# Two heads' short rows beneath one another, one transpose each, and loads of v that wait for ScalarE

## The reference

```
B, H, S, D = 4, 8, 576, 64
scores = matmul(q, k.T) / sqrt(D)                      # per batch and head, 576 x 576
kth    = 32nd largest of each row
attn   = softmax(where(scores >= kth, scores, -1e9))
x      = matmul(attn, v)  -> rows (B*S, H*D) = (2304, 512)

h = x @ w_in; g = max(h, 0) + alpha * min(h, 0); x = g @ w_out     # 512 -> 2048 -> 512

live = x @ w_skip > 0;  e = argmax(x @ w_gate)                     # 8 experts
out  = x;  out[live] = x + gate * (max(x @ w1[e], 0) @ w2[e])      # 512 -> 1024 -> 512
```

## Time and profile before

| what | us |
|---|---|
| time, median of 3 runs | 1122.45 |
| the profiled execution, its time | 1120.2 |
| its span, first to last instruction | 1118.4 |
| DVE busy | 907.7 (81%) |
| PE busy | 924.3 (83%) |
| ACT busy | 631.6 (56%) |
| POOL busy | 427.6 (38%) |

### The profile page before, as it was taken

One profiled execution on the slowest core, in us unless ns is written; L12 is line 12 of the kernel. 1 busy time (PEld: TensorE's weight loads), 2 busy tenths in 40 slices (PEclk: granted clock), 3 DMA queues, 4 the chain that ended last, 5 costly groups with the idle time before them and its releaser, 6 DMA issues.

```text
span 1118.4 us, 22555 instructions
## 1 busy us (share of the span) xinstructions
PE 924.3 (83%) x6271; PEld 616.4 (55%) x6272; DVE 907.7 (81%) x2006; ACT 631.6 (56%) x1324; POOL 427.6 (38%) x598
## 2 busy tenths in 40 slices
PE   5345588898899889988988898889888898399996
PEld 2223356575667566665756576657565666243342
DVE  4899999999999999999999999999999451711110
ACT  3785869637954784588458746964784371110100
POOL 0136647612841483068127702851384000201110
PEclk9986679999999999999999999999999799699999
DMA  7910201004001300220031003100300156735750
GB/s 205 369 34 3 51 22 33 23 2 119 8 21 50 78 0 21 75 53 10 11 96 32 21 1 101 26 22 16 81 1 1 43 191 224 237 100 180 226 197 18
DMA packets 98658, 84.05 MB, mean 75 GB/s; under 512 B 69116, under 2 KB 77308, under 8 KB 98048
## 3 DMA queue, kind: packets, MB, share of 16 engines
q1 hardware_dynamic: 94544, 78.56, 23.3%
q0 software_dynamic: 1488, 3.15, 0.8%
q10 hardware_dynamic: 2528, 1.18, 0.4%
HBM read 72.64 MB, written 11.53 MB: 75 GB/s over the span
## 4 chain that ended last, share of the span: by engine, by line
PE 55%; issue 10%; POOL 10%; ACT 9%; DMA 7%; DVE 5%; SPq 1%; POOLq 1%; ACTq 0%; DVEq 0%
PE acc L607 16%; PE acc L574 8%; PE sc L545 7%; PE acc L593 6%; DMA arena<-in_moe_w_dram 5%; PE pt_full L563 5%; POOL pos_part L361 4%; POOL arena L363 2%; PE sc L715 2%; PE pt_full L775 2%; POOL arena L1330 2%; PE acc L616 2%; ACT arena L847 2%; DVE best L1053 1%; PE acc L622 1%
## 5 line engine op out<-in xcount | busy, mean ns | idle before, releaser
L1053 DVE MAX8 best<-arena 128x8 f32<-128x576 f32 x576 | 403.5, 741 | 9.6 <-issue 5.4
L1066 DVE MATCH_REPLACE8 arena<-best,arena 128x576 f32<-128x576 f32 x432 | 315.8, 738 | 0.0
L1330 POOL TENSOR_SCALAR arena<-arena,row_inv 128x576 f32<-128x576 f32 x144 | 105.5, 750 | 360.0 <-DVE row_inv L1083 360.0
L593 PE MATMUL acc<-arena 128*128 (+1 forms) x1536 | 202.4, 286 | 28.0 <-ACT neg_part L886 26.1
L607 PE MATMUL acc<-arena 128*128 128x288 f16 x1536 | 202.0, 288 | 2.9 <-issue 2.9
L593 PEld LDWEIGHTS acc<-arena 128*128 128x128 f16 x1536 | 146.3, 98 | 78.9 <-issue 39.1
L607 PEld LDWEIGHTS acc<-arena 128*128 128x128 f16 x1536 | 149.5, 99 | 49.5 <-issue 12.9
L563 PE MATMUL pt_full<-ident,arena 128*128 128x128 f32 x576 | 101.9, 305 | 63.8 <-ACT arena L860 31.0
L838 ACT ACTIVATE arena<-sc 128x576 f32<-128x576 f32 x144 | 92.1, 642 | 86.1 <-PE sc L545 69.6
L1071 DVE SCALAR_TENSOR_TENSOR arena<-arena,best 128x576 f32<-128x576 f32 x144 | 128.0, 935 | 3.5 <-ACT arena L847 3.5
L563 PEld LDWEIGHTS pt_full<-ident,arena 128*128 128x128 f32 x576 | 72.7, 154 | 94.0 <-issue 51.0
(11 more groups left out here) (173 smaller groups left out, 942.1 us busy)
## 6 DMA issues: line engine op xcount, KB each, us to landing
arena<-in_moe_w_dram SPq DMA_DIRECT2D x64, 512.0 KB
nat<-in_v_dram SPq DMA_DIRECT2D x64, 128.0 KB, 2.2
nat<-in_k_dram SPq DMA_DIRECT2D x60, 128.0 KB, 2.7
x_rows<-x2n SPq DMA_DIRECT2D x24, 192.0 KB, 2.5
out_dram<-x2n SPq DMA_DIRECT2D x24, 192.0 KB, 2.6
nat<-in_q_dram SPq DMA_DIRECT2D x64, 64.0 KB, 2.1
arena<-in_moe_w_in_dram SPq DMA_DIRECT2D x4, 1024.0 KB, 7.3
arena<-in_moe_w_out_dram SPq DMA_DIRECT2D x4, 1024.0 KB, 13.7
```

The costliest lines, as they stand in the source:

```text
L593: last = nc.tensor.matmul(dst[:, 0:HALF], win16[:, a, d, f * P:(f + 1) * P], xT16[:, bass.ds(row + d, 1), b, :].rearrange("p b s -> p (b s)"),
L1053: nc.vector.max(best[:, gp, j, r, :], src).then_inc(max_found if r == 0 else dve_step, 1)
L1066: nc.vector.match_replace(left[:, j, :], best[:, gp, j, r, :], src, MASKED).then_inc(dve_step, 1)
L1330: nc.gpsimd.tensor_scalar(probs[:, gp, j, :], probs[:, gp, j, :], row_inv[:, gp, j:j + 1], 1.0, ALU.mult, ALU.mult)\
```

## The change

The four short rows of a quad's heads are no longer side by side in 32 (or 64) partitions. The second head pair's rows lie in the partitions beneath the first pair's: `q_rest` becomes 64 partitions of 128 numbers, `k_rest` 128 partitions of 128. One transpose each then gives the same 64 and 128 columns in the same bank. Each of the two loads becomes two DMAs of half the size, one for each head pair, so a pass's q and k come in 12 DMAs and not 10. The semaphore `pv_done`, with TensorE's wait for its own product, is gone; SyncE waits instead until ScalarE has rounded both halves of x of that pass, which it does after it has read the product.

```
-        k_rest = sb("k_rest", [REST, QUAD, D])
+        k_rest = sb("k_rest", [TWO * REST, TWO * D])
...
-        q_rest = arena[0:QREST, at[4]:at[5]].rearrange("p (h d) -> p h d", h=QUAD)
+        q_rest = arena[0:TWO * QREST, at[4]:at[5]]
...
-        DMAS_QK, DMAS_V = 2 * (QUAD + 1), QUAD + 1
+        DMAS_QK, DMAS_V = 2 * (QUAD + TWO), QUAD + 1
...
-            engine.dma_start(k_rest[:, :, :], quad_of(k, p)[:, FULL * P:S, :].rearrange("h r d -> r h d")).then_inc(qk_loaded, 16)
+            for c in range(TWO):
+                engine.dma_start(k_rest[c * REST:(c + 1) * REST, :].rearrange("r (h d) -> r h d", d=D),
+                                 quad_of(k, p)[2 * c:2 * c + 2, FULL * P:S, :].rearrange("h r d -> r h d")).then_inc(qk_loaded, 16)
...
-                    sp.wait_ge(pv_done, p - 1)
+                    sp.wait_ge(x_hi_ready, TWO * (p - 1))
...
-                    sp.wait_ge(pv_done, PASSES_A)
+                    sp.wait_ge(x_hi_ready, TWO * PASSES_A)
...
-                for c in range(TWO):
-                    nc.tensor.transpose(dst[:, c * QREST:(c + 1) * QREST], q_rest[:, 2 * c:2 * c + 2, :].rearrange("p h d -> p (h d)"),
-                                        ident[0:QREST, 0:QREST])
-                    o = TWO * QREST + c * REST
-                    last = nc.tensor.transpose(dst[:, o:o + REST], k_rest[:, 2 * c:2 * c + 2, :].rearrange("p h d -> p (h d)"), ident[0:REST, 0:REST])
-                last.then_inc(acc_ready, 1)
+                nc.tensor.transpose(dst[:, 0:TWO * QREST], q_rest[:, :], ident[0:TWO * QREST, 0:TWO * QREST])
+                nc.tensor.transpose(dst[:, TWO * QREST:TWO * (QREST + REST)], k_rest[:, :], ident[:, :]).then_inc(acc_ready, 1)
...
-                pe.wait_ge(acc_ready, items.base + items.used)
-                pe.sem_inc(pv_done, 1)
```

More of the change, by code:

```diff
@@ L381, in load_q @@
                       .then_inc(qk_loaded, 16)
[L382 removed]
+            for c in range(TWO):
+                engine.dma_start(q_rest[c * QREST:(c + 1) * QREST, :].rearrange("r (h d) -> r h d", d=D),
+                                 quad_of(q, p)[2 * c:2 * c + 2, bass.ds(first + QFULL * P, QREST), :].rearrange("h r d -> r h d")).then_inc(qk_loaded, 16)
         def load_k(engine, p):
```

5 lines of the change are left out of this document (2 added, 3 removed).

## The result

The changed kernel took 1137.91 us in the median of six runs (1127.98 to 1142.91); the kernel before, in six runs beside it, 1123.51 us (1120.51 to 1124.91). The ratio is 1.0112, 95% interval 1.0078 to 1.0146. The forecast was 1119.6 us with a range to 1123.2. A ratio leaves out the runs that are more than 1.5% above the fastest of their kernel, and a median doesn't, so the two can differ.

The account below looks back on a forecast made before the run. Two nearly level chains of waits bound the loop, VectorE's and TensorE's, the latter later by 0.34 us a step. Median 1122.45 with -2.7 - 0.6 + 0.4 = -2.9 gives 1119.6 us; own range 1118.4 to 1121.3, 8 in 10 1117.3 to 1123.2.

Parts of the forecast that it names:

- the sum itself: Whole kernel: -2.7 (waits) - 0.6 (second effect) + 0.4 (start) = -2.9 us, giving 1119.6 us for a median.
- the rivals: Whole kernel: VectorE untouched, 0.25; full 4.2 us gained, 0.17; late second load, 1134 us, 0.03; more masked sums met, 0.07.
- Four transposes into two: Short-row transposes in `prep`: 0.40 us instead of 0.77, of which ScalarE's copy lets 0.26 per `prep` arrive.
- TensorE's wait for its own product: Between `pv` and `prep`'s first transpose: 0.47 us go, but just 0.04 arrive, as ScalarE rounds x first.
- What VectorE lets through: Loop: VectorE's waits shrink by 2.7 us, plus 0.6 from a second effect (1.5 faster to 3.5 slower).
- the ring through `prep`: Loop: TensorE's chain of waits, period 105.83 us, was taken as later than VectorE's by 0.34 us a step.
- the wait of 1.06 us: VectorE's longest wait at a masked sum, in step 1: to fall by one `prep`, 0.30 us.
- Two more DMAs: Per pass: nothing lost in the loop; at the start 0.4 us slower (0.4 faster to 1.5 slower).
- One sign of being wrong: Loop: TensorE waiting for q and k before `prep` would show the forecast wrong; no size given.
- At the start: Before the loop: added issues 0.6 and split first load 0.2 slower, first `prep` 0.4 faster; 0.4 us slower.
- Later waits for v and the experts' weights: SyncE released 1.1 to 1.2 us later for v loads and experts' weights: costs nothing.
- the cover of 14.8 us: Experts' weights: SyncE's 14.8 us wait for TensorE covers the later start and shortens by about 1.

Follow-up runs that it names:

- dve_pad2: The changed kernel with two small VectorE reciprocals more per pass, results unread: 1135.1 us, ratio 1.0095.
- padw2: The changed kernel with two 128x128 transpositions more behind each preparation's last wait: 1133.7 us, ratio 1.0066.
- plus12: The changed kernel with 12 instructions more (long-fulfilled waits) on TensorE's queue behind the last routing: 1137.5 us, ratio 1.0091.
- before_again: The kernel before, unchanged, profiled a second time: one run, 1126.5 us.
- split_loads: The kernel before with only the short rows of q and k loaded in two DMAs each: 1130.1 us, ratio 1.0033.
- before_fill_last: The kernel before with seven unread 448-column products around the routing products in the last step alone: 1126.9 us, ratio 1.0027.
- after_fill: The changed kernel with seven unread 448-column products around the routing products in each loop step: 1126.4 us, ratio 1.0025.
- dve_pad: The changed kernel with one small VectorE reciprocal more per pass, result unread: 1139.7 us, too scattered for a ratio.
- my first padding experiments: The changed kernel with the short k rows' transposition doubled, or one or two transpositions added behind the preparation's last wait: 1137.4, 1133.3 and 1133.7 us.
- after_again: The changed kernel, unaltered, profiled a second time: one run, 1131.8 us.
- before_fill: The kernel before with seven unread 448-column products around the routing products in each loop step: 1123.8 us, ratio 1.0004.
- sync_only: The kernel before with only the waits changed (TensorE's own-product wait gone, SyncE waiting for rounded x); four transposes, ten loads: 1125.1 us, ratio 1.0035.
- plus30: The changed kernel with 30 instructions more (long-fulfilled waits) on TensorE's queue behind the last routing: 1131.5 us, ratio 1.0053.

## Why the prediction was wrong

**The step that failed is the sum itself.** Every duration in it was taken at an unchanged clock, and TensorE's granted clock stood neither among the terms nor among the rivals. Yet the row for the step showed it, 0.98 and not 1.00. That was one fall of 3.4 us per step, which cost the kernel 0.2 us at most and left no mark that one would notice in the chain of waits. In its place the runs showed four stretches of 13.7 us in the profile of the changed kernel, each in a step of 109.3 to 109.4 us for 105.8. Four times 3.5 us, less the 1.1 us by which its loop began earlier, make the 13.1 us that it loses up to `pv` 15, against a forecast gain of 2.9.

Over the seventeen profiles without wide products in the loop there are 102 such stretches. The 78 of 3.4 us begin 1.83 to 2.99 us behind the start of the routing products, and the 24 of 13.7 us begin 3.02 to 3.27 behind it; there is no exception on either side. It is no bound in general: in the last step, where other work follows, stretches of 13.7 us also came with the fall at 2.73, 2.74 and 2.95 us (dve_pad2, padw2, plus12). Steps with the former take 105.45 to 105.94 us, with the latter 109.30 to 109.64. `pv` 15 starts at 889.3 to 890.3 us with none of them in before, before_again, split_loads and before_fill_last (887.3 and 887.7 in the two with less work), at 892.8 to 894.3 with one, at 896.6 to 898.5 with two, at 900.0 with three and at 903.1 and 903.5 with four: 3.4 to 3.9 us each in the mean. That is the loss in the loop, and after_fill takes it away. The Trainium skill (TensorE: Matmul & The Clock Gate, Part 1) says that the gate runs freely and doesn't start with the kernel, so that transitions come at other places from run to run; before and before_again agree, 2.7 and 1.9 us.

Why the change brings the falls to the bad side follows in good part from their distance of 105.81 us. before's step of 105.83 us happens to be nearly the same, so its falls stand still; the changed kernel's of 105.57 lets them move 0.24 us later in each step, and some step of the six comes over 3 us. What stays open is where the first fall of the loop stands: 2.74 and 1.90 us in two executions of before, 3.23 and 2.64 in two of after. Nor was it found that restoring the length restores the time (dve_pad, dve_pad2).

**Four transposes into two.** As forecast locally: 0.20 apart, the copy 0.27 nearer (0.26 forecast). The pair itself was put too short: by the timeline it takes 0.53 us to its last end (594.30 to 594.83) and not 0.40, for 0.82 of the four, so 0.29 us are saved on TensorE and not 0.37. Its worth on the path was not as forecast: see below, on what VectorE lets through.

**TensorE's wait for its own product.** It went, and as forecast nearly nothing arrived: TensorE then waits 0.19 us for ScalarE's rounding of x ahead of its second group, and the copy starts 0.35 behind that rounding (0.38 before).

**What VectorE lets through.** Wrong. The prediction said that VectorE waits for another engine only at its masked sums. It also waits for 1.04 to 1.30 us at a search in every step, and the view of waits of the kernel before has these rows:

```profile
DVE best L1053 <- issue: 5.4, 5, 1.1
DVE best L1053 <- ACT arena L838: 4.2, 3, 1.5
```

Five of these waits stand under "issue", which names no engine and which I passed over; three are put down to ScalarE's stored scores by name, and these I missed as well. So the ring through `prep` was not the later one: both waits stayed (0.31 and 1.06 us), of the 2.4 us of waits forecast to go in the later steps 0.02 to 0.03 us a step went, and the short step's 0.26 us are nearly all VectorE's busy time, 104.45 to 104.20. Without falls even this is gone. The same error made my first padding experiments fail. What makes the scores come 1.06 us late is not shown. In step 1 the wait of 1.06 us is gone in the profile of after, as forecast, but this says nothing: at that place before_again waits 2.18 us and after_again 2.17.

**Two more DMAs.** In the loop no time was lost by them, but the margin is gone: the second half of the short k rows is issued at 479.9 us, lands 2.2 later, and the transposes start at 482.3. One sign of being wrong, TensorE waiting for q and k before `prep`, did appear: once in after, in its last step (where before_again waits 0.79 us too, with ten loads), three times for 0.2 to 0.3 us in after_again, and in after_fill in each step from the second of the loop on, 1.16 to 1.81 us where before_fill waits 0.49 to 0.96. One row each of after and after_fill:

```profile
807.01 0.66 PE L519 MATMUL acc<-ident,nat 128*128 128x128 f32 x4 [0.78 <-DMA k_rest<-in_k_dram]
580.95 0.63 PE L519 MATMUL acc<-ident,nat 128*128 128x128 f32 x4 [1.43 <-DMA k_rest<-in_k_dram]
```

after_fill's steps are 105.54 to 105.75 us all the same, which says again that this path has room. At the start the sign was wrong, by luck. VectorE's release by the weights' scales came at 44.34 us and not at 45.02, 0.7 earlier, although each half costs SyncE the price of a whole issue (0.64 and 0.61 us for k), and the way from its first load of the second pass to the weights grew by the upper bound of 1.1 us. What came earlier were the first eight score products, in before, after and after_again:

```profile
12.50 2.29 PE L545 MATMUL sc<-kT,qT 64*128 64x288 f32 x8 [0.48 <-ACT kT L829]
11.98 1.24 PE L544 MATMUL sc<-kT,qT 64*128 64x288 f32 x8 [0.48 <-ACT kT L825]
12.13 2.29 PE L544 MATMUL sc<-kT,qT 64*128 64x288 f32 x8 [0.48 <-ACT kT L825]
```

The granted clock is 1.00 there in after; in the other two its records begin later. With the slow products after_again releases VectorE at 46.38 us, 1.4 us later than before did, so at an equal pace the start is slower, as forecast.

**Later waits for v and the experts' weights.** Nothing, as forecast. But the cover of 14.8 us is 15.1 and not a microsecond less, and 15.0 in sync_only; why is not shown.

**The part behind the loop** was no term at all. The six profiles with four transposes and no wide products took 227.4 to 234.4 us there (mean 230.6), the ten with merged ones 229.8 to 240.3 (mean 235.5). This difference of 5 us goes with more stalls on issue, 6.4 us for 3.7 in the mean. The tie is loose: before_fill takes 239.8 us with 3.1 of stalls, plus30 229.8 with 4.7. Near three of after's five stalls the clock is low for 3.4 us. A page of the Trainium skill (Runtime: NRT & Kernel Launch, Instruction fetch mechanics) holds that a taken branch to instructions not yet fetched stalls its engine. The stalls do sit in the experts' branches, but of after's five only the one at 1078.7 us has a branch instruction just ahead of it in the trace, and two (1097.5 and 1121.4) fall in the middle of a group of transposes. That the places of the instructions are the cause is supported by one pair of runs and not shown; it stays open.

## What to carry over

When a profile's granted clock is below 1.00 in a stretch, find the fall and what TensorE did ahead of it before forecasting anything: a harmless stretch became four times as long from a shift of 0.3 us, and one such stretch cost more than ten times the 0.26 us that the edit saved in a step. A wait listed under "issue" belongs in the balance of an engine as much as one with a name. And when two rings look level, add idle work to the one believed to be late and see whether the period moves; that was the cheapest test of the forecast's main step. A third: compare two executions of the same kernel before a difference of a few microseconds is put down to an edit.

## What the runs showed of the hardware

- In the loop the clock came back either after 3.4 us or after 13.7, with 0.02 us in the place of the fall between the two (2.99 and 3.02 us behind the start of the routing products); in the last steps after 3.4, 6.8, 10.2 or 13.7.
- The next fall came 105.81 us after one with a short stretch and 109.23 after one with a long stretch, in steps of 105.45 to 105.94 and of 109.30 to 109.64 us alike.
- The stretch of 3.4 us behind the routing products cost 0 to 0.2 us in a step although TensorE's clock was at half in it, and VectorE was never idle in the one shown above; 20.8 us behind them one cost 1.4 us.
- With seven products of 448 columns before and among the 24 of nine columns the clock stayed at 2.4 GHz over them and for 17 us or more behind them, in the loops of two kernels; with five it fell at about 3 us in two of six stretches.
- Halves of a small DMA cost their issuing queue as much as the whole, 0.62 us each for k, and land in 2.2 us instead of 2.6.
- The part behind `pv` 15 differed by 6 us between two executions of the same kernel (228.4 and 234.4 us, 238.0 and 231.6), and its first eight score products by 1.05 us (1.24 and 2.29).
